# One fill of transposed probabilities a step, and the products with V two steps later, in a kernel of attention, MLP and experts

## The reference, cut to what matters

```python
scores = scale * q @ k.T                      # 4 batches x 8 heads, 576 tokens, head size 64
scores = where(causal, -1e9, scores + cum[i] - cum[j])   # cum: running sum of log f
attn = exp(scores - rowmax(scores))
attn = attn / (sum(attn) + 1e-9)
x = attn @ v                                  # then (2304, 512)
h = x @ w_in; g = piecewise(h); y = g @ w_out # 512 -> 2048 -> 512
out = routed experts of y                     # 8 experts, 512 -> 1024 -> 512
```

## Time and profile before

| | us |
|---|---|
| median of three executions | 889.11 |
| lowest and highest | 887.54, 890.61 |
| the profiled execution | 887.77 |
| its span | 885.8 |
| first score to last score of attention | 12 to 211 |

### The profile page before, as it was taken

How to read it: one execution, slowest core, us unless ns; L and a number is a source line. 1 busy time by engine, 2 the same in 40 slices (tenths; PEclk the granted TensorE clock), 3 DMA queues, 4 the chain that set the end, 5 groups by cost and what they waited for, 6 DMA issues and landing times.

```text
span 885.8 us, 13981 instructions
## 1 busy us (share of the span) xinstructions
PE 849.2 (96%) x5138; PEld 803.8 (91%) x5139; DVE 413.8 (47%) x1001; ACT 395.0 (45%) x906; POOL 366.4 (41%) x370
## 2 busy tenths in 40 slices
PE   4999999999989999999999999999999999999995
PEld 3888888888889999999999999999998998998984
DVE  3777788886555544444444444454424211210201
ACT  4777777776656534534434434443432111221211
POOL 7765787784555411201201020064411493010294
PEclk9999999999999999999999999999999999999998
DMA  5666888872200211021021021432143254213040
GB/s 180 191 202 205 254 253 254 259 228 78 55 1 1 72 54 54 16 97 41 27 98 54 28 99 38 135 123 68 36 132 96 96 168 141 64 55 119 30 142 26
DMA packets 66334, 94.58 MB, mean 107 GB/s; under 512 B 6662, under 2 KB 42502, under 8 KB 66256
## 3 DMA queue, kind: packets, MB, share of 16 engines
q1 hardware_dynamic: 58160, 79.43, 29.5%
q10 hardware_dynamic: 6336, 9.44, 3.0%
q0 software_dynamic: 1760, 4.72, 1.4%
HBM read 69.82 MB, written 24.27 MB: 106 GB/s over the span
## 4 chain that ended last, share of the span: by engine, by line
PE 88%; ACT 5%; DVE 4%; issue 1%; POOL 1%; DMA 0%; SPq 0%; ACTq 0%; POOLq 0%
PE psum L1370 23%; PE psum L1371 22%; PE psum L1372 22%; PE psum L1345 6%; PE psum L1304 6%; PE psum L1329 4%; PE psum L1310 1%; DVE ptl L1000 1%; ACT xo L798 1%; DVE g L1029 1%; ACT pth L792 1%; PE psum L1425 1%; PE psum L1424 1%; ACT pr L783 1%; ACT hpos L829 1%
## 5 line engine op out<-in xcount | busy, mean ns | idle before, releaser
L1370 PE MATMUL psum<-xh,winh 128*128 128x384 f32 x384 | 133.1, 347 | 3.6 <-ACT hpos L829 3.6
L1371 PE MATMUL psum<-xl,winh 128*128 128x384 f32 x384 | 131.6, 343 | 0.0
L1372 PE MATMUL psum<-xh,winl 128*128 128x384 f32 x384 | 131.6, 343 | 0.0
L1370 PE MATMUL psum<-gh,wouth 128*128 128x384 f32 x384 | 128.7, 335 | 0.0
L1371 PE MATMUL psum<-gl,wouth 128*128 128x384 f32 x384 | 128.4, 334 | 0.0
L1372 PE MATMUL psum<-gh,woutl 128*128 128x384 f32 x384 | 128.3, 334 | 0.0
L829 ACT ACTIVATE hpos<-psum,minus 128x384 f32<-128x384 f32 x96 | 55.9, 582 | 154.6 <-DVE hclip L1026 154.3
L1029 DVE TENSOR_TENSOR g<-hpos,hsq 128x384 f32<-128x384 f32 x96 | 66.3, 690 | 112.0 <-ACT hsq L831 112.0
L622 POOL TENSOR_TENSOR xst<-xst 128x384 f32<-128x384 f32 x24 | 24.6, 1024 | 183.3 <-DMA xst<-rinv_d 183.2
L783 ACT ACTIVATE pr<-pr,mmin 128x64 f32<-128x64 f32 (+2 forms) x144 | 81.7, 568 | 38.0 <-DVE mmin L984 38.0
L1142 DVE SCALAR_TENSOR_TENSOR hl<-psum,hh 128x384 fp32r<-128x384 f32 x48 | 26.8, 557 | 140.9 <-ACT hh L860 140.9
(11 more groups left out here) (216 smaller groups left out, 1937.1 us busy)
## 6 DMA issues: line engine op xcount, KB each, us to landing
praw<-moe_w SPq DMA_DIRECT2D x48, 256.0 KB, 2.7
...
```

Source lines behind the costliest of these rows:

```text
L1370: nc.tensor.matmul(psum_at, ah, bh, start=start, stop=False)
L1371: nc.tensor.matmul(psum_at, ah, bl, start=False, stop=False)
L1372: return nc.tensor.matmul(psum_at, al, bh, start=False, stop=stop)
```

## The change

The eight fills of a pair get steps of their own: k = 0 to 7 are turned at steps 1, 3, 5, 6, 7, 8, 9 and 11 counted from the pair's first, that is, the last two at steps 0 and 2 of the next pair (table `WHEN`). The fills of all pairs are numbered in time (`nth_fill`), and the two PSUM banks alternate by that number; all waits that counted fills count by it. `high` and `low` still stand one step behind. `attend_early` moves from step 6 to 7, `attend_late_a` from step 2 to 4, `attend_late_b` from step 4 to 5 of the next pair; their copies are DVE's at steps 5 and 6 (3 and 5 before) and ACT's at step 8 (7 before). The turn of the last inverse moves from step 145 to 147. The places of `up_block(0)`, `up_block(1)`, `hidden(0)` and `hidden(1)` stay. No instruction is added or dropped.

```diff
--- before.py
+++ after.py
@@ -55,7 +55,7 @@
     NG = 4
     STEPS = NB * PAIRS
     AHEAD = 4
-    TAIL = 6
+    TAIL = 7
     ROW = 5 * P
     SIDE = 6 * P
     FILLS = 8
@@ -97,8 +97,22 @@
             return i * P if b == 0 else (i + 2) * P
         return SIDE + (ROW * b + (i - 4) * P if b < 4 else 3 * ROW)
 
-    def fills_of(i):
-        return [k for k in range(FILLS) if FILL[k][0] == i]
+
+
+    WHEN = (1, 3, 5, 6, 7, 8, 9, 11)
+    ORDER = sorted(((p, k) for p in range(PAIRS) for k in range(FILLS)), key=lambda pk: NB * pk[0] + WHEN[pk[1]])
+
+    def fills_at(n):
+        return [(p, k) for p, k in ORDER if NB * p + WHEN[k] == n]
+
+    def nth_fill(p, k):
+        return ORDER.index((p, k))
+
+    def inverse_bank(p):
+        return (4, 5)[nth_fill(min(p + 1, PAIRS - 1), FILLS - 1) % 2]
+
+    def last_fill(i):
+        return max(k for k in range(FILLS) if FILL[k][0] == (i | 1 if i < 8 else 8))
 
     with ExitStack() as ctx:
         def sem(name):
@@ -360,9 +374,9 @@
             full = tile[:, at:at + P]
             return bass.AP(full.tensor, full.offset, [[full.ap[0][0], P], [ROW, nb], [1, ni * P]])
 
-        def of_bank(k):
+        def of_bank(p, k):
             _, b, nb, i, ni = FILL[k]
-            full = psum[:, PT[k % 2], 0:nb * ni * P]
+            full = psum[:, PT[nth_fill(p, k) % 2], 0:nb * ni * P]
             return full if nb == 1 or i < 4 else full.rearrange("p (b c) -> p b c", b=nb)
 
         @block.sync
@@ -438,7 +452,7 @@
                 if i == 5 and p < PAIRS - 2:
                     load_qk(p + 2)
                     load_v(p + 2)
-                if i == 5 and 0 <= p - 1 < PAIRS:
+                if i == 6 and 0 <= p - 1 < PAIRS:
                     store_x(p - 1)
                 if i == 7 and p < PAIRS - 2:
                     load_c(p + 2)
@@ -784,12 +798,12 @@
                                      accum_out=rsum[:, p % 2, i:i + 1]).then_inc(exped, 1)
 
             def high(p, k):
-                act.wait_ge(turned, FILLS * p + k + 1)
+                act.wait_ge(turned, nth_fill(p, k) + 1)
                 if k == 0 and p >= 1:
                     act.wait_ge(early, p)
                 if k == 2 and p >= 1:
                     act.wait_ge(late_b, p)
-                nc.scalar.copy(stacked(pth, k), of_bank(k)).then_inc(pt_h, 1)
+                nc.scalar.copy(stacked(pth, k), of_bank(p, k)).then_inc(pt_h, 1)
 
             def copy_early(p):
                 act.wait_ge(early, p + 1)
@@ -811,15 +825,13 @@
                 act.wait_ge(wo_in_s, 16 * (f_ + 1))
                 nc.scalar.copy(wouth[:, f_, :], woraw[:, f_, :]).then_inc(wo_h, 1)
 
-            for n in range(-AHEAD, STEPS + 1):
+            for n in range(-AHEAD, STEPS + 4):
                 if 0 <= n + 2 < STEPS:
                     exp(n + 2)
-                p, i = tile_of(n - 1)
-                if 0 <= n - 1 < STEPS:
-                    for k in fills_of(i):
-                        high(p, k)
+                for p, k in fills_at(n - 1):
+                    high(p, k)
                 p, i = tile_of(n)
-                if i == 7 and 0 <= p < PAIRS:
+                if i == 8 and 0 <= p < PAIRS:
                     copy_early(p)
                 if p - 1 in X_LOADED and i == 1:
                     split_x(X_LOADED.index(p - 1))
@@ -970,7 +982,7 @@
                     dve.wait_ge(zero_ok, 2)
                 dve.wait_ge(scored, n + 1)
                 if p >= 1:
-                    dve.wait_ge(turned, FILLS * (p - 1) + max(fills_of(i | 1 if i < 8 else 8)) + 1)
+                    dve.wait_ge(turned, nth_fill(p - 1, last_fill(i)) + 1)
                 if p >= 2 and i == 0:
                     dve.wait_ge(exped, NB * (p - 1))
                 bank = (10 * p + i) % 4
@@ -996,14 +1008,14 @@
                 nc.vector.reciprocal(rinv[:, p % 2, 0:NB], rden[:, p % 2, :]).then_inc(inv_ok, 1)
 
             def low(p, k):
-                dve.wait_ge(pt_h, FILLS * p + k + 1)
-                nc.vector.tensor_tensor(stacked(ptl, k), of_bank(k), stacked(pth, k).bitcast(F32),
+                dve.wait_ge(pt_h, nth_fill(p, k) + 1)
+                nc.vector.tensor_tensor(stacked(ptl, k), of_bank(p, k), stacked(pth, k).bitcast(F32),
                                         ALU.subtract).then_inc(pt_l, 1)
 
             def copy_turned(p):
                 if p >= 2:
                     dve.wait_ge(r_out[p % 2], 16 * (p // 2))
-                nc.vector.tensor_copy(rturn[:, p % 2, :], psum[0:NB, PT[1], P:2 * P]).then_inc(r_copied, 1)
+                nc.vector.tensor_copy(rturn[:, p % 2, :], psum[0:NB, inverse_bank(p), P:2 * P]).then_inc(r_copied, 1)
 
             def copy_late_a(p):
                 dve.wait_ge(late_a, p + 1)
@@ -1034,22 +1046,20 @@
             for n in range(-AHEAD, STEPS + TAIL):
                 if 0 <= n + 3 < STEPS:
                     masked(n + 3)
-                p, i = tile_of(n - 1)
-                if 0 <= n - 1 < STEPS:
-                    for k in fills_of(i):
-                        low(p, k)
-                    if i == 8 and p >= 1:
+                for p, k in fills_at(n - 1):
+                    low(p, k)
+                    if k == FILLS - 1 and p >= 1:
                         copy_turned(p - 1)
                 p, i = tile_of(n)
                 if i == 7 and 0 <= p < PAIRS:
                     denominator(p)
                 if i == 8 and 0 <= p < PAIRS:
                     invert(p)
-                if i == 3 and 0 <= p - 1 < PAIRS:
+                if i == 5 and 0 <= p - 1 < PAIRS:
                     copy_late_a(p - 1)
-                if i == 5 and 0 <= p - 1 < PAIRS:
+                if i == 6 and 0 <= p - 1 < PAIRS:
                     copy_late_b(p - 1)
-                if p == PAIRS and i == 1:
+                if p == PAIRS and i == 3:
                     dve.wait_ge(turned, FILLS * PAIRS + 1)
                     copy_turned(PAIRS - 1)
                 if p - 1 in X_LOADED and i == 1:
@@ -1318,15 +1328,16 @@
                 if k == 0 and p == 0:
                     pe.wait_ge(zero_ok, 2)
                 pe.wait_ge(exped, NB * p + last + 1)
-                if FILLS * p + k >= 2:
-                    pe.wait_ge(pt_l, FILLS * p + k - 1)
-                if k == 1 and p >= 2:
+                bank = PT[nth_fill(p, k) % 2]
+                if nth_fill(p, k) >= 2:
+                    pe.wait_ge(pt_l, nth_fill(p, k) - 1)
+                if k == 2 and p >= 2:
                     pe.wait_ge(r_copied, p - 1)
                 x = None
                 for b in range(b0, b0 + nb):
                     for i in range(i0, i0 + ni):
                         at = (b - b0) * ni + i - i0
-                        x = nc.tensor.transpose(psum[:, PT[k % 2], at * P:(at + 1) * P],
+                        x = nc.tensor.transpose(psum[:, bank, at * P:(at + 1) * P],
                                                 pr[:, at_tile(i) + b * P:at_tile(i) + (b + 1) * P], ident[:])
                 if k == FILLS - 1 and p >= 1:
                     x = turn_inverse(p - 1)
@@ -1334,7 +1345,7 @@
 
             def turn_inverse(p):
                 pe.wait_ge(inv_ok, p + 1)
-                return nc.tensor.transpose(psum[:, PT[1], P:2 * P], rinv[:, p % 2, :], ident[:])
+                return nc.tensor.transpose(psum[:, inverse_bank(p), P:2 * P], rinv[:, p % 2, :], ident[:])
 
             def head(p, h, i0, ni, dst, signal):
                 todo = [(m, b) for m in (pth, ptl) for b in range(KB) if 2 * b < i0 + ni]
@@ -1348,7 +1359,7 @@
                     x.then_inc(signal, 1)
 
             def attend_early(p):
-                pe.wait_ge(pt_l, FILLS * p + 2)
+                pe.wait_ge(pt_l, nth_fill(p, 1) + 1)
                 pe.wait_ge(vsplit, p + 1)
                 if p >= 1:
                     pe.wait_ge(x_late_b, p)
@@ -1356,7 +1367,7 @@
                 head(p, 1, 0, 4, psum[:, PX, 4 * D:8 * D], early)
 
             def attend_late_a(p):
-                pe.wait_ge(pt_l, FILLS * (p + 1))
+                pe.wait_ge(pt_l, nth_fill(p, FILLS - 1) + 1)
                 if p >= 1:
                     pe.wait_ge(x_late_a, p)
                 head(p, 0, 4, 5, psum[:, PY, 0:5 * D], late_a)
@@ -1390,19 +1401,18 @@
             for n in range(-AHEAD, STEPS + TAIL):
                 if 0 <= n + AHEAD < STEPS:
                     score(n + AHEAD)
+                for p, k in fills_at(n):
+                    turn(p, k)
                 p, i = tile_of(n)
-                if 0 <= n < STEPS:
-                    for k in fills_of(i):
-                        turn(p, k)
                 if n in UP_EARLY:
                     up_block(UP_EARLY.index(n))
-                if i == 6 and 0 <= p < PAIRS:
+                if i == 7 and 0 <= p < PAIRS:
                     attend_early(p)
-                if i == 2 and 0 <= p - 1 < PAIRS:
+                if i == 4 and 0 <= p - 1 < PAIRS:
                     attend_late_a(p - 1)
-                if i == 4 and 0 <= p - 1 < PAIRS:
```

(3 more changed lines are left out.)

## The result

The changed kernel takes 899.1 us (median of four executions, 897.59 to 899.49) beside 888.5 for the kernel before on the same chip (four executions, 887.54 to 890.61, one more than the table above has); the ratio is 1.0109, with an interval of 1.0093 to 1.0126. It is slower by 10.6 us by the medians, and by 11.1 by the profiled executions (898.91 beside 887.77). The forecast was slower by 7.4, that is 896.5, with a range of 891.5 to 901.

The account below looks back on a forecast made before the run. PE, busy 96% of the span, was taken as the bound, so only its gaps could move. Terms -1.5 + 3.2 + 5.4 + 0.4 - 0.7 + 0.6 = +7.4 us gave 896.5 us on the median's scale, range 891.5 to 901.

Parts of the forecast that it names:

- the clock: Behind PE's new gap at the seam: work at 1.2 GHz costs between 0 and 1.7 us; taken as +0.6 us.
- the eight intervals with `combine_x`: POOL's pairs 7 to 14: period 13.08 instead of 12.68 us, +3.2 us in all.
- the seam: From the last `late_b` to `up_block(2)`: PE idles some 5 us behind `hidden(0)`'s chain on DVE and ACT, +5.4 us.
- the six ordinary intervals: Pairs 0 to 4 and the last: old bank gap exchanged for smaller ones, -0.25 us each, -1.5 us in all.
- the returned waits: Behind the seam: earlier waits of `up_block(3)` and (4) for ACT's part of `hidden` partly go, -0.7 us.
- (c): The forecast's own case: gaps at fill 4, POOL loop, 5 us at the seam; 892 to 900 us, chance 0.60.
- POOL's loop: Pairs with `combine_x`: chain from `late_b` through POOL's `ql`, score and fill 2 back to `late_b` takes 13.08 us.
- The lower bound of 12.8: Pairs with `combine_x`: without DVE's x work meeting `ql`, the loop is 12.8 us and the eight sum to +0.8.
- The gap at fill 4: Each pair: ACT's rounding of fill 2 waits for `late_b`, so PE waits 0.66 us for that bank.
- rival (a): Attention pairs: no gap at fill 4, no binding POOL loop, old gap goes; -4.8 us, 884.3 us; chance 0.03.
- Rival (f): As (c), but the low clock lies over work alone, full 1.7 us paid instead of 0.6; 897.6 us, chance 0.18.
- rival (d): DVE slips in the pairs, or clock falls again or in later layers (1.7 us each); 901 to 905 us, chance 0.09.

Follow-up runs that it names:

- Experiment 3: Changed kernel with POOL's `combine_x` on 64 of 384 columns in attention; total 991.97 us, not comparable; period 13.08 to 12.65 us in four of eight pairs.
- Experiment 2: Changed kernel with `attend_late_b` back at step 4, ahead of fill 2, and its copy at step 5; 899.17 us, ratio 1.0119.
- experiment 6: Changed kernel with `late_b` at step 4, `attend_early` one step earlier, `hidden` and the splits of x on ACT and DVE one step later; 881.85 us, ratio 0.9922.
- experiment 1: Changed kernel with `hidden(0)` and `hidden(1)` one step later on DVE, behind the last remainder; 892.65 us, ratio 1.0049.
- experiment 4: Changed kernel with 24 never-read products on PE in the idle gap at the seam, ahead of the last inverse's waits; 895.35 us, ratio 1.0077.
- 7: As experiment 6, but the splits of x on ACT and DVE stay at step 1; 889.61 us, ratio 1.0005.
- 8: As experiment 6, with ACT rounding a fill ahead of the step's exponential instead of behind it; 879.87 us, ratio 0.9888.
- 5: Kernel before with only the products with V and their copies moved as in the changed kernel, fills as before; 897.28 us, ratio 1.0095.

## Why the prediction was right, and where its sum was off

**The sign and its mechanisms held.** The range held the time, and so did "slower". Without the clock, the terms sum to 6.8 us in the forecast and to 6.6 in the traces. That the two agree so well is partly luck: the eight intervals with `combine_x` and the seam came as forecast, but the six ordinary intervals gave -2.3 instead of -1.5 and the returned waits -1.2 instead of -0.7, against +0.9 at `up_block(5)` to (7), a term that the forecast did not have. And the bounds of (c), 889.11 + 5.1 + 3.3 + 1.1, add up to 898.6, not to the 900 written there; the 899.1 lies above them, inside the wider range of 891.5 to 901.

**POOL's loop: right, to the hundredth.** Forecast 13.08 us for the eight pairs with `combine_x`, measured 13.04 to 13.09, PE's score 0.10 us behind `ql` in each and POOL idle for 2.52 before `vv`. Experiment 3 shows it as a cause: less work in the loop, a shorter period. The lower bound of 12.8, "if `ql` undisturbed", was wrong in kind: `ql` is undisturbed (2.67), but DVE's split of x now meets `kl` (1.77 instead of 1.42 to 1.44), and the loop has the same length. A collision that moves from one instruction of a chain to its neighbour leaves the chain as long as it was.

**The gap at fill 4: right in size, half right in cause.** Forecast 0.66, measured 0.53; the ordinary pairs gain 0.32 (forecast 0.25). In the changed kernel ACT does wait for `late_b` (the row at 136.31 above). But the text treated that wait as what makes the gap, and rival (a) as what happens without it. Experiment 2 takes the wait away and the gap stays: two fills 1.5 us apart by their bank, with 0.95 us of PE's work in between. The general statement ahead of it, that one fill and one score a step cover 1.6 us, was wrong at this place, where the tiles of the next pair are at their smallest and fill 3 has two blocks only. It takes a product between the fills, as in experiment 6.

**The seam: right.** A gap of 5 us was forecast for 222 to 228 us, behind `hidden(0)`, and 4.92 us until 226.85 were found. Moving `hidden` (experiment 1) takes 3.3 of them away.

**Returned waits: undersized.** Forecast -0.7 from the idle times of the earlier trace rows; measured -1.2. Those idle times count from modelled ends, which reach some 0.2 into a gap; by starts they are 225.56 - 222.72 - 2.17 = 0.67 and, against 4.16 in the changed kernel, 0.46.

**The clock: the mis-sized term.** Forecast +0.6 net, bounds 0 and 1.7; measured +4.5. Two things went wrong. The price was read from the one stretch that the profile of before shows behind a gap of 2 us (about 3.4 us long), and then discounted because part of it might lie in idle time. Behind the longer gap the stretch was 6.8 us long (226.54 to 233.37) and lay nearly whole over work: 3.0 us by the rows above, 2.9 by experiment 4 from the inverse to the end of `up_block(2)`, and 3.4 to 3.7 with what followed from it. Rival (f), that work pays in full, pointed the right way but had the same too small price. The Trainium skill, "TensorE: Matmul & The Clock Gate", section "HAM oscillation — how this bites in real kernels", says that the burst behind a long wait starts at half rate; this trace agrees (0.50 from 226.99 to 231.89, behind 4.92 us), and experiment 4, where there is no such wait, has 1.00 there. The price is not fixed by the gap, though: experiment 3 has the same gap of 4.92 us, and there the stretch is 3.4 us long and the late products take 4.21 us instead of 4.90. The second is the fall at 670 us, +3.2, which rival (d) named with 1.7 as its price.

**What stays open** is when the clock falls without a gap. The traces show what PE did before: 24 products of 8 and 16 columns for a router (666.56 to 669.15 at the last of them in the changed kernel). Each kernel has six such blocks. Of the 60 in the ten traces, 45 have a fall that begins about their end (from 0.2 us before it to 1.6 behind), four in the kernel before and five in the changed one. Every other fall between 30 and 870 us begins in a gap of PE of 1.6 us or more, or within 1.7 us behind one. But neither decides it. At the last block the stretch is 6.8 us long in the changed kernel and in experiments 4, 6 and 7, 3.4 in 1, 2 and 8, and there is none in the kernel before and in 3 and 5. PE's gap of 1.8 to 2.0 us in the first layer precedes a fall in the kernel before and in 2, 5 and 7, and none in the changed kernel and in 1, 3, 4, 6 and 8. The gap of 1.61 us at the seam has a fall behind it in 7 and none in 1, 6 and 8. No run moved the router's work or one of these gaps alone. Some 3 us of any comparison here depend on it.
